# ScalarE writes gate times sigmoid(gate) itself, in a chain of attention, a gated layer and a layer of four experts

## The reference

```python
xn = x / rms * rms_g
g = xn @ w_gate
silu = g * (1.0 / (1.0 + np.exp(-g)))
val = xn @ w_val
x = silu * val @ w_out
```

## Time and profile before

| | |
|---|---|
| median of 3 runs | 890.36 us (890.15 to 891.17) |
| the profiled execution | 892.34 us, its span 890.5 us |
| TensorE busy | 845.5 us, 95% of the span, 4816 matmuls |
| VectorE | 532.7 us, 60%, 835 instructions |
| ScalarE | 249.6 us, 28%, 490 instructions |
| GpSimd | 407.8 us, 46%, 432 instructions |

### The profile page before, as it was taken

One profiled execution on the slowest core, in us unless ns is written; L12 is line 12 of the kernel. 1 busy time (PEld: TensorE's weight loads), 2 busy tenths in 40 slices (PEclk: granted clock), 3 DMA queues, 4 the chain that ended last, 5 costly groups with the idle time before them and its releaser, 6 DMA issues.

```text
span 890.5 us, 12801 instructions
## 1 busy us (share of the span) xinstructions
PE 845.5 (95%) x4816; PEld 776.9 (87%) x4816; DVE 532.7 (60%) x835; ACT 249.6 (28%) x490; POOL 407.8 (46%) x432
## 2 busy tenths in 40 slices
PE   6987899999999999759999999999999999999998
PEld 5765799999999999648889989889998989989897
DVE  3696766766666667965455454545545455554545
ACT  2666323232222223242222222222222222222211
POOL 3494682736455446770382533553353255335100
PEclk9998899999999999969999999999999999999999
DMA  9711010010101001000110111011011101101003
GB/s 344 281 53 47 1 46 26 24 48 25 48 24 48 25 13 60 24 24 1 42 54 9 40 49 48 1 48 48 1 48 48 48 1 48 48 1 48 25 0 142
DMA packets 12875, 43.58 MB, mean 49 GB/s; under 512 B 1552, under 2 KB 1552, under 8 KB 12816
## 3 DMA queue, kind: packets, MB, share of 16 engines
q1 hardware_dynamic: 12816, 42.77, 13.6%
HBM read 39.62 MB, written 3.15 MB: 48 GB/s over the span
## 4 chain that ended last, share of the span: by engine, by line
PE 88%; DVE 6%; issue 3%; ACT 2%; DMA 1%; SPq 0%; DVEq 0%
PE bank L478 28%; PE bank L479 28%; PE bank L480 28%; PE bank L460 2%; PE bank L418 1%; DVE x_lo L231 1%; DVE x_sum L227 1%; DVE x_all L819 1%; DMA ring<-qkv 1%; PE bank L438 1%; DVE hid L879 1%; PE bank L450 1%; PE bank L431 0%; DVE gate L865 0%; ACT h_hi L674 0%
## 5 line engine op out<-in xcount | busy, mean ns | idle before, releaser
L478 PE MATMUL bank<-x_hi,w_hi 128*128 128x384 f32 x784 | 266.2, 340 | 20.2 <-ACT m L661 10.4
L480 PE MATMUL bank<-x_lo,w_hi 128*128 128x384 f32 x784 | 264.9, 338 | 0.0
L479 PE MATMUL bank<-x_hi,w_lo 128*128 128x384 f32 x784 | 264.9, 338 | 0.0
L931 DVE SCALAR_TENSOR_TENSOR out_acc<-bank,p_norm,out_acc 128x512 f32<-128x512 f32 x180 | 134.9, 750 | 130.1 <-PE bank L480 129.9
L478 PEld LDWEIGHTS bank<-x_hi,w_hi 128*128 128x128 f32 x784 | 148.9, 190 | 29.4 <-issue 23.1
L479 PEld LDWEIGHTS bank<-x_hi,w_lo 128*128 128x128 f32 x784 | 148.9, 190 | 5.4
L480 PE MATMUL bank<-wd_lo,h_hi 128*128 128x512 f32 x384 | 151.9, 396 | 0.0
L479 PE MATMUL bank<-wd_hi,h_lo 128*128 128x512 f32 x384 | 151.7, 395 | 0.0
L478 PE MATMUL bank<-wd_hi,h_hi 128*128 128x512 f32 x384 | 149.7, 390 | 0.0
L480 PEld LDWEIGHTS bank<-x_lo,w_hi 128*128 128x128 f32 x784 | 148.7, 190 | 0.0
L328 POOL TENSOR_TENSOR w_lo<-w_raw,w_hi 128x256 fp32r<-128x256 f32 x196 | 146.1, 781 | 2.3
(11 more groups left out here) (69 smaller groups left out, 936.2 us busy)
## 6 DMA issues: line engine op xcount, KB each, us to landing
w_raw<-wu SPq DMA_DIRECT2D x28, 512.0 KB, 4.3
ring<-qkv SPq DMA_DIRECT2D x24, 512.0 KB, 7.5
wd_raw<-wd SPq DMA_DIRECT2D x22, 512.0 KB, 3.5
out<-out_acc SPq DMA_DIRECT2D x12, 256.0 KB, 2.0
decay_mask<-t_decay_mask SPq DMA_DIRECT2D x1, 512.0 KB, 5.2
y_decay<-t_y_decay SPq DMA_DIRECT2D x1, 256.0 KB, 7.7
small_sb<-small SPq DMA_DIRECT2D x1, 32.0 KB, 4.9
```

Of the source, the lines that this page charges most:

```text
L478: pe.matmul(dst, s_hi, m_hi, start=first, stop=False, skip_group_check=True)
L479: pe.matmul(dst, s_lo, m_hi, start=False, stop=False, skip_group_check=True)
L480: return pe.matmul(dst, s_hi, m_lo, start=False, stop=last, skip_group_check=True)
L931: nc.vector.scalar_tensor_tensor(out=to, in0=new, scalar=p, in1=to, op0=ALU.mult, op1=ALU.add).then_inc(posted, 1)
```

## The change

ScalarE's two activations of a unit use the function Silu, which is the gate times its sigmoid, in place of Sigmoid. VectorE's product `gated` is left out, all 48 of them. The semaphores `sig_ready` and `gated_ready` become one, `silu_ready`, which ScalarE raises; `hidden` on VectorE and M1 and M2 on TensorE wait for it.

```diff
             def product(q, c, j, k, name):
                 if name == "M1" and 2 <= q < Q1 + 2:
-                    pe.wait_ge(gated_ready, 2 * (q - 2) + 2)
+                    pe.wait_ge(silu_ready, 2 * (q - 2) + 2)
...
                 elif name == "M2" and 2 <= q < Q1 + 2:
-                    pe.wait_ge(gated_ready, 2 * (q - 2) + 1)
+                    pe.wait_ge(silu_ready, 2 * (q - 2) + 1)
...
-            def sigmoid(q, a):
+            def silu(q, a):
                 s = q % 2
                 if a == 0:
                     act.wait_ge(c11_ready, q + 1)
-                    nc.scalar.activation(gate[:, s, 0, :], bank[3 * s + 2][:, 0:TB], ACT.Sigmoid).then_inc(sig_ready, 1)
+                    nc.scalar.activation(gate[:, s, 0, :], bank[3 * s + 2][:, 0:TB], ACT.Silu).then_inc(silu_ready, 1)
                 else:
                     act.wait_ge(up_done, up_count(q, "M4"))
-                    nc.scalar.activation(gate[:, s, 1, :], bank[3 * s][:, 0:TB], ACT.Sigmoid).then_inc(sig_ready, 1)
+                    nc.scalar.activation(gate[:, s, 1, :], bank[3 * s][:, 0:TB], ACT.Silu).then_inc(silu_ready, 1)
...
-            def gated(q, a):
-
-                s = q % 2
-                dve.wait_ge(sig_ready, 2 * q + a + 1)
-                nc.vector.tensor_tensor(gate[:, s, a, :], bank[3 * s + (0 if a else 2)][:, 0:TB], gate[:, s, a, :],
-                                        ALU.mult).then_inc(gated_ready, 1)
-
             def hidden(q, a):
                 s, slot = q % 2, q % SLOTS1
-                dve.wait_ge(gated_ready, 2 * q + a + 1)
+                dve.wait_ge(silu_ready, 2 * q + a + 1)
...
                 some(1)
-                gated(q, 0)
                 c22_sum(q)
                 some(2)
-                gated(q, 1)
                 hidden_all(q)
```

More of the change, by code:

```diff
@@ L197, in build @@
         c12_ready = sem("c12_ready")
-        gated_ready = sem("gated_ready")
-        sig_ready = sem("sig_ready")
+        silu_ready = sem("silu_ready")
         hid_ready = sem("hid_ready")
@@ L681, in unit1 @@
                 copy_up(q, "M6", u2)
-                sigmoid(q, 0)
+                silu(q, 0)
                 copy_up(q, "M7", u3)
-                sigmoid(q, 1)
+                silu(q, 1)
                 hidden_hi(q, 1)
@@ L733, in _ @@
             copy_up(0, "M7", u3)
-            sigmoid(0, 0)
-            sigmoid(0, 1)
+            silu(0, 0)
+            silu(0, 1)
             copy_up(1, "M1", m1)
@@ L742, in _ @@
             part_hi(1, "A22")
-            sigmoid(1, 0)
+            silu(1, 0)
             copy_up(1, "M7", u3)
             part_hi(1, "S3")
-            sigmoid(1, 1)
+            silu(1, 1)
             part_hi(1, "S4")
@@ L1015, in _ @@
             sum_of(1, "S2")
-            gated(0, 0)
-            gated(0, 1)
             hidden(0, 1)
@@ L1026, in _ @@
             hidden_lo(0, 0)
-            gated(1, 0)
-            gated(1, 1)
             hidden_all(1)
```

## The result

The changed kernel took 882.11 us (median of 4, 881.14 to 883.12) against 890.25 us (median of 4) of the kernel before: 8.14 us less, a ratio of 0.9907 with a 95% interval of 0.9890 to 0.9925. Measured again on another chip the ratio was 0.9907 (0.9888 to 0.9926). The forecast was 884.4 us with a range of 881.0 to 888.2; the gain of 5.9 us was too small by 2.2.

What follows compares the result with a forecast made beforehand. The prediction took TensorE as the bound, gaining only at stops behind products: 1.04 + 1.05 + 1.24 + 2.36 + 0.23 = 5.92 us off the median of 890.36 gives 884.4 us, range 881.0 to 888.2.

Steps and rivals of the forecast that it cites:

- The bound and the places: First gated layer: TensorE bounds; gain only where it stops behind a product, at the start, four pairs and unit 4.
- C: Rival, ScalarE: Silu takes two passes, 984 ns, leaving 2.5 to 3.7 us gain; 0.14 shared with another rival.
- E: Rival, ScalarE: Copy and Silu share no table, so loads make it slower, about 908 us; 0.05 with other slowdowns.
- D: Rival: TensorE's stops hang on something the profile doesn't name, so Silu removes nothing there, 890.4 us; chance 0.08.
- First stop, 1.04: Start, before M7 of unit 1: without two products hidden(0,1) and the chain behind it come 1.04 us earlier.
- Second stop, 1.05 + 1.24: Start, before M6 of unit 2: 1.05 us from two products, 1.24 from hidden(1,1) starting before GpSimd's x_lo.
- cap: Start, M6 of unit 2: TensorE itself ready at 97.81 us, so at most 3.98 us gained there.
- rival A: Start and middle: h_lo pairs slip ahead of GpSimd, or clock stays up; 7.9 to 8.6 us off, chance 0.13.
- The middle, 2.36: Four pairs of units: both stops together, 1.11 us, shrink by 0.59 each time with the same contention, 2.36 us.
- the band that got 0.60: The forecast's own band, whole kernel: 4.5 to 7.5 us off, 882.9 to 885.9 us, chance 0.60.
- The small one, 0.23: At 124.97 us: a matmul starts 0.40 us after the one before instead of 0.17; same chain, uncontended, 0.23 us.
- The rule of the lock: Start, hidden(1,1): GpSimd and two-input VectorE operations lock the port pair for a whole instruction; basis of the 1.24 us.

Runs made afterwards that it cites:

- e4: Changed kernel with the product put back in units 2 to 23 for the first half of the tokens only, written into the bank: 883.05 us, ratio 0.9915.
- e6: Kernel before with Silu in place of Sigmoid and all products kept: 890.23 us, ratio 0.9991.
- e7: Kernel before, all products kept, GpSimd's sums of odd weight blocks held until VectorE's h_lo are done: 886.75 us, ratio 0.9949.
- e11: Kernel before with its products, GpSimd's sums held off and two copies moved ahead in ScalarE's order at the start: 882.01 us, ratio 0.9932.
- e1: Changed kernel with all 48 products put back, written into the bank: 892.69 us, 1.0032 of the kernel before.
- e3: Changed kernel with the products put back in units 2 to 23, written into the bank: 888.55 us, 0.9986 of the kernel before.
- e10: Changed kernel with the products put back in units 2 to 23 in their old form, written into the gate tile: 887.88 us, ratio 0.9987.
- e9: Changed kernel with the products put back in units 0 and 1 in their old form, written into the gate tile: 886.56 us, ratio 0.9969.
- e2: Changed kernel with the products put back in units 0 and 1 only, written into the bank: 887.72 us, ratio 0.9977.

## Why the prediction was right, and where its sizes were off

- *The bound and the places.* Right: TensorE's two stops at the start, the four pairs and unit 4. The 14 matmuls at the pairs and at unit 4 hold 4.44 of the middle's 4.51 us. e4 and the unchanged end of the layer (the stop before the last half's down tiles is 1.61 us after, 1.63 before) show the products off the path to be worth nothing.
- *A Silu costs a sigmoid, one load.* Right: 492 ns and one load of 1283 ns in the trace, e6 at 0.9991. Rivals C and E are out, and so is D: the stop before M6 of unit 2, put down to "issue", moved with the chain. The Trainium skill, "ScalarE: Activation LUTs", section "Table sets: the hidden batching unit", says that copy is in every set and that only a change of set is paid. The trace agrees: copies of `L660` run between the Silus with no further load.
- *First stop, 1.04.* Measured 1.07 (88.19 against 89.88, less the 0.62 by which that execution was early).
- *Second stop, 1.05 + 1.24.* Measured 3.92 with the first, where 3.33 was forecast. Both terms are right in their place: `hidden(1,1)` fell from 1.80 to 0.54 us. The missing 0.59 is the clock. Behind the stop of 3.82 us TensorE was at 1.2 GHz from 90.3 us on, in M7 of unit 1; behind the shorter one M7 ran at 2.4 GHz to its end (0.34 us a matmul at 89.14) and only M4 and the first three of M3 were at the lower level. M7's end releases a copy, that `x_hi` of S3, that GpSimd's two operations, and these `hidden(1,1)`. The prediction had named this as help towards a cap and had it in rival A; in its sum the term was missing. The table on M7 bears it out: without M7's time the products of units 0 and 1 cost 3.3 to 3.5 us of start in every profile, the 3.33 of the forecast, and what the clock adds changes from execution to execution, from 0.1 to 1.0 us. That it was 0.59 in the two profiles compared is in part luck. The stop before M6 is still 1.41 us, not under one as forecast, since TensorE is there earlier too.
- *The middle, 2.36.* The step "with the contention the same both stops together (1.11) shrink by 0.59" failed: the pairs gave 1.09, 1.01, 0.93 and 1.11 us, 4.14 in all. The contention was not the same. `hidden` met another part of GpSimd's sums and took 0.65 instead of 1.16 us, so `h_lo` started 1.1 us earlier against TensorE, not 0.59, and the two of them, unchanged at 2.75 us, then fit. e7 shows that without this meeting there are no stops, products or not. Rival A had the outcome (7.9 to 8.6 off; it was 8.1), with a chance of 0.13, while the band that got 0.60 ended at 7.5 off. Of its two conditions the clock helped. The other, the first `h_lo` slipping ahead of `w_hi`, came true in all four pairs (by 0.44 to 0.46 us), but not what A drew from it: the second `h_lo` then stood behind `w_hi`, and the two together ended no sooner after their start.
- *The small one, 0.23.* TensorE has no stop at M6 of unit 4 any more. It gave 0.31: the second matmul behind a stop also starts 0.25 us after the first instead of 0.17, and this 0.08 was left out here and at the first stop of each pair. Those stops were not all alike either (0.28, 0.18, 0.20, 0.28).
- *The rule of the lock.* The Trainium skill's "SBUF — State Buffer", section "SBUF: two separate sides", says that the one that starts first has the port pair for its whole instruction. The rows of unit 22 agree: `hidden` 0.05 us ahead of `w_hi` took 0.56 us (before, e6, e7, e11), 0.01 to 0.02 us behind it about 2.1 (e1, e3, e10), and this was worth 1.43 us there.

## What to carry to other kernels

Busy time taken off an engine is worth what it takes off the stops of the bound engine: here 26.5 us of VectorE gave 8.1, and 22 of the 48 products (12 us of work) gave nothing. Where a chain meets another engine's work, as VectorE's met GpSimd's here, the plain shift is a poor guess: 0.59 us off the chain gave 0.9 to 1.1 us in the four pairs, and 1.05 us gave 2.3 at the second stop of the start. Such a term should be bounded from where the other engine's operations begin and end relative to the chain. Before an operation is removed, look whether a stop is a queue order or a meeting: one added wait on an engine with time in hand gave about half of this change's gain.

## What the runs showed of the hardware

- A VectorE operation that reads two SBUF tiles (0.56 us alone) took 2.10 us when it started in the same hundredth of a microsecond as GpSimd's `w_hi` (e10), and 0.56 when 0.05 us ahead; then GpSimd's took 2.08 instead of 1.71.
- Such an operation of VectorE, started inside one of GpSimd's, ended 0.39 to 0.42 us after the end of that one: behind the 1.81 us of `x_lo`, the 0.74 of a sum, and the 1.71 and 1.89 of `w_hi`.
- TensorE behind the first long stop of the start, in the six matmuls of M7: behind 2.73 to 2.76 us of standing all at full clock in four executions, the lower level from the fifth on in one (e4); behind 3.78 to 3.91 us the lower level from the first (e6, e7), third (before, e9) or fourth (e1, e2). So a longer stop mostly went with an earlier fall, but its length alone doesn't fix the place: it was 3.82 us both before and in e7. Behind the second stop no fall came after 2.58 to 2.87 us, and ten matmuls at the lower level after 3.19 (e6, e7). In the kernel before the clock stayed down until 97.0 us, in the changed one until 92.8; the granted clock of 90 to 100 us rose from 0.66 to 0.85.
- An added semaphore wait in front of a VectorE operation that was already satisfied cost 0.06 us of start (0.65 against 0.59 us after the start of the product before it, at all 22 places of e10).
